# Four small buffers moved from the middle to the end of the on-chip allocation, in a fused attention and MoE kernel on one core

## The reference

```python
# decayed linear attention: batch 2, 8 heads, 768 positions, head dimension 64, in blocks
intra = (q @ k.T * Dmask) @ v;  inter = (q * lam_pow) @ kv_state
kv_state = lam_block * kv_state + (k * rev_pow).T @ v
# MoE on 1536 tokens: model 512, 4 experts of width 1024, every expert for every token
p = domain_probs / domain_probs.sum(-1)
x1 = sum over e of p[:, e] * (relu(x @ w1[e]) @ w2[e])
# second MLP: width 2048
h = x1 @ w_in;  out = (h * cos(h)) @ w_out
```

## Time and profile before

| | us |
|---|---|
| median of 3 runs | 843.71 (843.05 to 845.42) |
| the profiled execution's own time | 845.39 |
| its span, first to last instruction | 843.6 |
| PE busy | 827.5 (98% of the span) |
| PEld busy | 764.2 (91%) |
| DVE busy | 578.1 (69%) |
| ACT busy | 291.2 (35%) |
| POOL busy | 235.8 (28%) |
| mean granted TensorE clock | 0.996 of full |

### The profile page before, as it was taken

How to read it: one execution, slowest core, us unless ns; L and a number is a source line. 1 busy time by engine, 2 the same in 40 slices (tenths; PEclk the granted TensorE clock), 3 DMA queues, 4 the chain that set the end, 5 groups by cost and what they waited for, 6 DMA issues and landing times.

```text
span 843.6 us, 12216 instructions
## 1 busy us (share of the span) xinstructions
PE 827.5 (98%) x4788; PEld 764.2 (91%) x4788; DVE 578.1 (69%) x1024; ACT 291.2 (35%) x552; POOL 235.8 (28%) x236
## 2 busy tenths in 40 slices
PE   7988999999999999999999999999999999999998
PEld 6878999999999999999999999997888888888886
DVE  6866667667667667667667667666777777777776
ACT  4543222222222222222222212246544445454542
POOL 4854433433432432432432433263000000000000
PEclk9999999999999999999999999999999999999999
DMA  9932111021011021011011010100110101010003
GB/s 324 314 118 74 30 35 38 26 76 38 26 38 38 25 75 38 26 38 38 26 38 33 31 38 28 36 26 17 34 35 29 38 26 37 27 38 26 1 0 150
DMA packets 19869, 44.88 MB, mean 53 GB/s; under 512 B 2344, under 2 KB 2392, under 8 KB 19812
## 3 DMA queue, kind: packets, MB, share of 16 engines
q1 hardware_dynamic: 19812, 44.10, 16.3%
HBM read 40.93 MB, written 3.17 MB: 52 GB/s over the span
## 4 chain that ended last, share of the span: by engine, by line
PE 90%; DVE 2%; ACT 1%; POOL 1%; issue 0%
PE ps L909 32%; PE ps L888 27%; PE ps L983 16%; PE ps L964 15%; POOL h_lo L402 0%; DVE temps L775 0%; POOL x_lo L394 0%; DVE temps L687 0%; DVE temps L771 0%; DVE temps L682 0%; ACT temps L564 0%; DVE w_lo L637 0%; DVE temps L714 0%; ACT temps L558 0%; ACT h_hi L503 0%
## 5 line engine op out<-in xcount | busy, mean ns | idle before, releaser
L402 POOL TENSOR_TENSOR h_lo<-temps,h_hi 128x384 fp32r<-128x384 f32 x128 | 135.7, 1060 | 317.7 <-ACT h_hi L503 317.7
L673 DVE TENSOR_TENSOR y<-ps,y 128x384 f32<-128x384 f32 x240 | 133.3, 555 | 110.4 <-PE ps L909 110.4
L503 ACT ACTIVATE h_hi<-temps 128x384 fp32r<-128x384 f32 x128 | 67.3, 525 | 378.5 <-DVE temps L687 378.5
L909 PE MATMUL ps<-h_hi,w_hi 128*128 128x384 f32 x512 | 174.7, 341 | 3.4 <-POOL h_lo L402 3.3
L909 PE MATMUL ps<-h_lo,w_hi 128*128 128x384 f32 x512 | 173.7, 339 | 0.0
L909 PE MATMUL ps<-h_hi,w_lo 128*128 128x384 f32 x512 | 173.1, 338 | 0.0
L888 PE MATMUL ps<-x_hi,w_hi 128*128 128x384 f32 x448 | 152.8, 341 | 2.9 <-ACT temps L516 1.8
L888 PE MATMUL ps<-x_lo,w_hi 128*128 128x384 f32 x448 | 152.9, 341 | 0.0
L888 PE MATMUL ps<-x_hi,w_lo 128*128 128x384 f32 x448 | 152.2, 340 | 0.0
L909 PEld LDWEIGHTS ps<-h_hi,w_hi 128*128 128x128 f32 x512 | 96.4, 188 | 8.1 <-issue 6.7
L909 PEld LDWEIGHTS ps<-h_hi,w_lo 128*128 128x128 f32 x512 | 96.5, 188 | 0.0
(11 more groups left out here) (82 smaller groups left out, 1108.0 us busy)
## 6 DMA issues: line engine op xcount, KB each, us to landing
w_raw<-w_in SPq DMA_DIRECT2D x96, 256.0 KB, 2.6
att<-att_in SPq DMA_DIRECT2D x24, 512.0 KB, 6.4
temps<-p_scr SPq DMA_DIRECT2D x4, 768.0 KB, 3.9
out<-y SPq DMA_DIRECT2D x12, 256.0 KB, 2.0
att<-dp_in SPq DMA_DIRECT2D x1, 24.0 KB
p_scr<-att SPq DMA_DIRECT2D x1, 24.0 KB
lam<-lam_in SPq DMA_DIRECT2D x1, 6.0 KB, 1.7
```

The costliest lines, as they stand in the source:

```text
L402: pool.tensor_tensor(hs_lo[:, s % 2, f, at], r_ring[:, n % R_RING, :], f32(hs_hi[:, s % 2, f, at]), ALU.subtract).then_inc(s_hlo, 1)
L503: act.activation(hs_hi[:, s % 2, f, CT * b:CT * (b + 1)], r_ring[:, n % R_RING, :], ACT.Copy).then_inc(s_hhi, 1)
L673: dve.tensor_tensor(at, from_bank, at, ALU.add).then_inc(s_y, 1)
L909: mm = pe.matmul(ps[:, DOWN_BANK + g % DOWN_BANKS, 0:CT], ww[:, s // SIDES % 2, f, at], hh[:, s % 2, f, tokens], start=(f == 0 and n == 0) ...
```

## The change

The four `sb` lines of `kpow`, `lam`, `dsum` and `first` move from before `w1_hi0` to behind `temps`.

```diff
         w_sum = sb("w_sum", [P, 4, FF2])
-        kpow = sb("kpow", [P, PAIRS, 2])
-        lam = sb("lam", [P, HEADS + PAIRS])
-        dsum = sb("dsum", [UNITS, P])
-        first = sb("first", [P, 1])
         w1_hi0 = sb("w1_hi0", [P, 7 * FF2], F32R)
         w1_lo0 = sb("w1_lo0", [P, 7 * FF2], F32R)
...
         temps = sb("temps", [P, 6912])
+
+        kpow = sb("kpow", [P, PAIRS, 2])
+        lam = sb("lam", [P, HEADS + PAIRS])
+        dsum = sb("dsum", [UNITS, P])
+        first = sb("first", [P, 1])
```

## The result

The changed kernel takes 832.04 us (median of 4 runs, 830.19 to 832.82), against 844.57 us (843.05 to 848.79) for the kernel before in the same comparison. The ratio is 0.9841, with a 95% interval of 0.98 to 0.9881: it is faster by 1.6%, a small change whose interval excludes 1. The forecast was 843.7 us and no change, with a range of 840.0 to 847.5 us.

The account below looks back on a forecast made before the run. The prediction took TensorE's matmul pitch in the MLP stages as the bound, with weight loads close behind in the MoE. All five parts were taken as 0, leaving the median of 843.71 at 843.7 us, range 840.0 to 847.5 us.

Parts of the forecast that it names:

- third rival: In TensorE's MLP matmuls, matching offsets of weights and moving data shorten the pitch: 822 us, or 839 for a tenth; 6%.
- parts 1 and 2: MLP matmuls: h's move as moving data (end +1.5 us) and w1's as weights (end -2.0 us), each taken as 0.
- First rival: In the MoE, TensorE's two reads collide at the same offset: 3 ns a matmul, 8.6 us slower, 852 us; 5%.
- Second rival: In attention's first 50 us, att loads lose DMA rate at 128 bytes past: middle +6, so 850 us; 6%.
- Parts 3 and 5: VectorE, ScalarE and GpSimd instructions at new offsets (first two at most 2 and 5 ns), and moved small buffers: 0 each.
- Fourth rival: After attention, half-clock stretches of 1.8 us each vanish or are added: 840.1 or 847.3 us; 4% to each side.

Follow-up runs that it names:

- mov256: Changed kernel with padding so that moving data (x, h) start 256 past a multiple of 512 bytes, weights (w1, w2) 128 past: 843.75 us, ratio 0.998.
- wts256: Changed kernel with padding so that weights (w1, w2) start 256 past a multiple of 512 bytes, moving data (x, h) 128 past: 842.96 us, ratio 0.9966.
- all0: Changed kernel with 384 bytes of padding ahead of the first buffer, so that all operands begin at multiples of 512 bytes: 832.11 us, ratio 0.9833.
- all256: Changed kernel with 128 bytes of padding ahead of the first buffer, so weights and moving data start 256 past a multiple of 512: 830.26 us, ratio 0.9816.
- small_mid_padded: Kernel before, small buffers left in place, 384 bytes of padding behind them so w1, att, h, y, temps start 128 past a multiple of 512: 831.54 us.
- per_line: Changed kernel with padding so that w2 and h start 256 past a multiple of 512 bytes, w1 and x 128 past: 834.78 us, ratio 0.9886.
- data_lo_plus128: Changed kernel with padding so that x_lo and h_lo start 256 past a multiple of 512 bytes, all else 128 past: 843.42 us, ratio 0.9972.

## Why the prediction was wrong

**The case and its price.** I gave the third rival, matching offsets relieve TensorE, 6% and two prices: 822 us if half of about 11 ns a matmul were the address, 839 if a tenth. A tenth is 1.1 ns and half is 5.5 ns. The measured gains are 2.5 ns in the MoE, between the two, and 6.3 ns in the second MLP, above both; 832 lies between the two times. The direction was right, but that the time fell between the prices was luck, for the sum took the gain from the part of a matmul that is not columns. By the same sum the pitches after the change give (226.1 - 174.7) / 128 = 0.40 ns per column and 20 ns beside it, where it was 0.43 and 11. So by the rival's own sum the cost was not in the part that the rival priced.

**The step that failed: parts 1 and 2.** I wrote that "the trace of before contains each operand's price at the new offset", and compared L888 with L909 as if each showed the price of one operand's place. But the price is one of a pair. Before the change L888 had moving data at 128 and weights at 256, and L909 the reverse. Each line held one mismatch of 128 bytes, so their equal 1.40 us showed only that a mismatch costs the same either way round, which mov256 and wts256 confirm at 843.75 and 842.96 us. In place of the zeros of the two parts, the runs show 2.5 ns for each of 2880 matmuls and 6.3 ns for each of 1152, about 14.5 us, and the measured time lies 8 us below the range. I named the pair as the one new thing in "What the change really does" and then summed zeros of single operands. The honest bound for the pair was open on both sides, and no MLP row of the kernel before could close it: all of them were mismatched.

**The argument against the third rival** was the same mistake. That L964 and L983 have opposite offsets and still the same 1.40 us is what the rival predicts as well.

**Weight loads as a bound.** I read the 446 of 450 us of load busy time as a sign that a slower read would show in the MoE, and that the second MLP had 45 us of cover. It was the other way round: the larger cost for each matmul was in the second MLP, 6.3 against 2.5 ns, with loads at 188 ns in both kernels. The busy time of a load did not show the cost; the interval between starts did.

**First rival, collision at equal offsets.** Its sign was wrong. Now that every MLP matmul has equal offsets, its loads take 188 to 189 ns, and attention's loads of the same 128x128 form, whose offsets were equal before and after, still take 191 ns:

```profile
L830 PEld LDWEIGHTS ps<-att 128*128 128x128 f32 x32 | 3.9, 191 | 0.5
```

So the 3 ns that the rival was built on do not come from a shared offset; where they come from, no run shows. The Trainium skill, page "SBUF — State Buffer", section "Who interferes with whom", gives TensorE two independent read ports, one for the moving operand and one for the weights. The trace agrees as far as equal offsets go, where nothing was lost. It does not agree at unequal ones: there the relative addresses of the two reads lengthen the pitch by up to 6.8 ns (226.1 to 232.9 ns at 32 bytes), and the measurement decides.

**Second rival, DMAs.** It did not occur: the share and rate of the first 20 us are 0.90 and 324 GB/s against 0.90 and 322. The page's DMA issues of the changed kernel, for the earlier trace rows:

```profile
w_raw<-w_in SPq DMA_DIRECT2D x96, 256.0 KB, 2.6
att<-att_in SPq DMA_DIRECT2D x24, 512.0 KB, 6.0
...
out<-y SPq DMA_DIRECT2D x12, 256.0 KB, 2.0
```

The landing of att is 6.0 us at 128 past, and 6.4 and 6.6 us in all0 and all256, where it begins at multiples of 256; but small_mid_padded, at 128 past too, has 6.4 us, and wts256, at 256, has 6.8 us. No run shows the charge that the Trainium skill's page "DMA: Bandwidth & Descriptors", section "How a descriptor splits into AXI transactions", sets for a start off 256 bytes, 0.2 us by my estimate; the spread between kernels is as large.

**Parts 3 and 5 held.** VectorE's and ScalarE's pairs are unchanged (L638 683 ns, L747 685, L450 618, L552 624), and the place of the small buffers is worth nothing (831.54 us without moving them).

**Fourth rival, the clock.** It stayed at two half-clock stretches after attention, of which these windows of the changed kernel show one each, and the mean clock at 0.996, so no part of the difference between the two profiled executions comes from it.

```profile
58.00:60.00 2.00, 2.00 (x8) 1.77 (x6) 0.56 (x1) 1.01 (x3) 0.85 (x2) 0.50 0.00 0
...
68.00:70.00 2.00, 2.00 (x8) 2.00 (x7) 0.56 (x1) 0.00 (x0) 1.92 (x4) 0.50 0.00 0
```

**The words of the change**, of which the prediction speaks, promise starts at multiples of 512 bytes. No operand begins at one after the change, as read from the addresses. It works because it makes offsets equal; all0, which does what the words say, takes 832.11 us and is no faster.

## What to carry to other kernels

Where TensorE is the bound, it is worth trying to lay out all matmul operands so that their starts have the same remainder by 256 bytes, weights and moving data alike, high and low parts alike; the small odd-sized buffers then go to the end or get padding. Shown is this for float32r matmuls of 384 and 512 columns in this one kernel; other types and shapes were not tried. Look at the interval between matmul starts, not at busy times: 2.5 to 6 ns of some 175 to 230 were 1.5% of the whole kernel. And when two groups of a trace cost the same, ask whether they differ in the thing that you want to price, or share it in mirror image.

## What the runs showed of the hardware that I had not expected

In this kernel TensorE's pitch depends on the difference of the start addresses of its weights and its moving data, modulo 256 bytes, at the differences tried (0, 32, 64, 128, 192, 256 and 384 bytes). In the second MLP a pitch of 226 ns becomes 232 to 233 ns at 32, 64 and 128 bytes, and 228.5 ns (215 us / 941) at 192. In the MoE 174.7 ns becomes 175.4 at 64 and 177.0 at 128, and stays at 32 and 192. A crossing from one offset to another lengthens the step after it too (by 3.2 ns in per_line), and in data_lo_plus128 the step before the odd matmul is the slowest (235.5 ns). In the differences tried, the address itself, 0, 128 or 256 past a multiple of 512, made no difference. By what part of the read path this comes about was not tested.
